# Block transposes of q and k on VectorE in place of TensorE transposes, in an attention and feed-forward kernel on one core

## The reference

```python
def _attn_ref(q, k, v, mem_k, mem_v):
    chunk, left_ctx, right_ctx = (32, 16, 8)
    scale = 1.0 / np.sqrt(D)
    for c in range(S // chunk):
        c_start = c * chunk
        c_end = c_start + chunk
        l_start = max(0, c_start - left_ctx)
        r_end = min(S, c_end + right_ctx)
        k_full = np.concatenate([mem_k, k[:, :, l_start:r_end]], axis=2)
        v_full = np.concatenate([mem_v, v[:, :, l_start:r_end]], axis=2)
        scores = scale * np.matmul(q[:, :, c_start:c_end], k_full.transpose(0, 1, 3, 2))
        scores = scores - np.max(scores, axis=-1, keepdims=True)
        a = np.exp(scores)
        a = a / (np.sum(a, axis=-1, keepdims=True) + 1e-09)
        out[:, :, c_start:c_end] = np.matmul(a, v_full)

def _moe_ref(x, w_in, w_out, g_ln):
    h = x @ w_in
    e = np.exp(h - np.max(h, axis=-1, keepdims=True))
    solu = h * e / (np.sum(e, axis=-1, keepdims=True) + 1e-09)
    ln = (solu - mean(solu)) / np.sqrt(var(solu) + 1e-06) * g_ln
    return ln @ w_out

def _moe2_ref(x, w_in, w_out):
    h = x @ w_in
    return (h * np.clip(h + 3.0, 0.0, 6.0) / 6.0) @ w_out
```

## Time and profile before

| | us |
|---|---|
| median of 3 runs | 904.52 |
| lowest, highest | 903.02, 905.22 |
| the profiled execution, its own time | 903.32 |
| its span, first to last instruction | 901.5 |
| mean granted TensorE clock | 0.992 |

### The profile page before, as it was taken

The page is one execution under the profiler, slowest core; times in us unless marked ns, Lnnn a source line. Parts: engine busy times, 40 slices in busy tenths (PEclk is TensorE's granted clock), DMA queues, the critical chain, the costliest instruction groups (busy, mean ns, idle before and its releaser), DMA issues.

```text
span 901.5 us, 18748 instructions
## 1 busy us (share of the span) xinstructions
PE 876.4 (97%) x7170; PEld 792.1 (88%) x7170; DVE 646.7 (72%) x1054; ACT 460.5 (51%) x1129; POOL 263.8 (29%) x308
## 2 busy tenths in 40 slices
PE   6899999999999999999999999999999999999998
PEld 5778988898888989899888888888799999999998
DVE  4768768787666778857685545554898887979784
ACT  5667555656565554537674555545754333333331
POOL 2474355465241453550122333223510000000000
PEclk8999999999999999999999999999999999999999
DMA  9965265554644474477733333333996434354341
GB/s 194 192 147 159 73 181 162 178 173 135 176 131 133 121 231 149 155 262 286 268 114 138 129 118 129 136 140 109 352 371 237 151 102 157 96 162 140 118 141 47
DMA packets 143496, 148.56 MB, mean 165 GB/s; under 512 B 91194, under 2 KB 102970, under 8 KB 142394
## 3 DMA queue, kind: packets, MB, share of 16 engines
q1 hardware_dynamic: 130272, 102.12, 37.3%
q0 software_dynamic: 7920, 38.94, 12.5%
q10 hardware_dynamic: 5226, 6.44, 2.2%
HBM read 89.92 MB, written 57.54 MB: 164 GB/s over the span
## 4 chain that ended last, share of the span: by engine, by line
PE 83%; DMA 5%; DVE 5%; ACT 3%; POOL 2%; issue 1%; SPq 1%; ACTq 0%; POOLq 0%; DVEq 0%
PE banks L1408 25%; PE banks L1147 25%; PE banks L1099 20%; PE banks L1114 3%; PE banks L1073 3%; PE banks L1044 2%; PE banks L991 2%; PE banks L1052 2%; PE banks L1090 2%; ACT prob L1497 1%; DMA xs_raw<-x_scratch 1%; POOL x_mix L897 1%; DMA x_mix<-x_scratch 1%; DMA x_mix_scratch<-x_mix 1%; DVE prob L1806 1%
## 5 line engine op out<-in xcount | busy, mean ns | idle before, releaser
L1408 PE MATMUL banks<-vs,gs 128*128 128x256 f32 x2016 | 242.8, 283 | 0.9 <-DMA vs<-v_split_scratch 0.8
L1408 PEld LDWEIGHTS banks<-vs,gs 128*128 128x128 f32 x2016 | 242.2, 192 | 1.6 <-DVE gs L1771 1.1
L1147 PE MATMUL banks<-xs,ws 128*128 128x512 f32 x1008 | 230.6, 390 | 0.5 <-ACT part L1550 0.2
L1147 PEld LDWEIGHTS banks<-xs,ws 128*128 128x128 f32 x1008 | 188.2, 188 | 41.6 <-issue 1.9
L1728 ACT CAST gs<-gs_raw 128x1792 fp32r<-128x1792 f32 x48 | 81.4, 1697 | 124.0 <-DVE gs_raw L2104 124.0
L1099 PE MATMUL banks<-y_t,w_out 128*128 128x384 f32 x768 | 141.1, 338 | 0.0
L1099 PEld LDWEIGHTS banks<-y_t,w_out 128*128 128x128 f32 x768 | 133.1, 188 | 0.8
L1099 PE MATMUL banks<-w_in,x_t 128*128 128x512 f32 x480 | 114.8, 395 | 1.1 <-DVE solu L1853 1.1
L1099 PEld LDWEIGHTS banks<-w_in,x_t 128*128 128x128 f32 x480 | 88.7, 188 | 19.9 <-DVE solu L1853 1.3
L2104 DVE TENSOR_TENSOR gs_raw<-gs_raw 128x256 f32<-128x256 f32 x192 | 82.2, 429 | 31.8 <-DMA gs_raw<-g_scratch 26.7
L1771 DVE TENSOR_TENSOR gs<-gs_raw,gs 128x1792 fp32r<-128x1792 f32 (+2 forms) x50 | 97.5, 1953 | 0.0
(11 more groups left out here) (104 smaller groups left out, 1012.7 us busy)
## 6 DMA issues: line engine op xcount, KB each, us to landing
g_scratch<-part SPq DMA_DIRECT2D x96, 256.0 KB, 2.0
gs_raw<-g_scratch SPq DMA_DIRECT2D x45, 512.0 KB, 4.0
x_scratch<-x_out ACTq DMA_DIRECT2D x32, 192.0 KB, 3.8
out_dram<-o_stage SPq DMA_DIRECT2D x11, 512.0 KB, 5.7
q_in<-in_q_dram SPq DMA_DIRECT2D x28, 192.0 KB, 3.0
v_split_scratch<-v_split POOLq DMA_DIRECT2D x3, 1792.0 KB, 7.6
ws<-w_split_scratch SPq DMA_DIRECT2D x21, 256.0 KB, 6.2
vs<-v_split_scratch SPq DMA_DIRECT2D x3, 1792.0 KB, 10.2
```

Source lines behind the costliest of these rows:

```text
L1147: mm = pe.matmul(ps, ws[:, W_OF[i], a, kc, :], xs[g][X_OF[i]][:, m, kc, :], start=(fresh and x == 0), stop=(x == len(passes) - 1), skip_gr ...
L1408: mm = pe.matmul(m_ps[i][:, s, :], gs[x][:, a, G_OF[i], s * P:(s + 1) * P], vs[p][:, m, V_OF[i], :], start=(p == 0 and s == 0 and y == 0), ...
```

## The change

Tiles 16 to 31 (batches 2 and 3) no longer have q and k turned by TensorE, and nothing is turned ahead in the first batch.

- **Relay.** While tiles 8 to 23 are worked on, SyncE issues eight DMAs a tile (`relay_step`), each from device memory to device memory. They put q and k of a group of four tiles into `q_blocks` and `k_blocks` so that each row of 128 partitions holds pieces of 32 floats of one 32-row chunk: 384 pieces of 128 bytes a DMA.
- **Loads.** A tile's q and k come from there, one DMA each, 384 bytes a run (`q_split`, `k_split`), behind a wait for the group's relay. In a batch's first tile twelve small DMAs bring the memory and left context rows as well.
- **VectorE.** `turn_blocks(n+1)` stands behind `norm_probs(n)`: three transposes of 32 by 32 squares (384, 256 and 128 columns), and one of 128 columns for `edge_t` in a batch's first tile. They write `q_t` and `k_t`.
- **ScalarE.** `join_blocks(n+1)` takes the place of the copies: three short copies within and between the k buffers, the second behind a wait for the first. The factor 1/8 moves into the exponential (`scale=SCALE`), whose bias is now `sbias`, one multiplication of the maxima per half tile, waited for.
- **TensorE.** The scores wait for `blocks_turned` and `qk_copied`; the probabilities' transposes of tiles 15 to 30 no longer wait for q and k copies.
- **GpSimd** waits for the first block's weights (`w_lo_done`) where it waited for `ahead_kept`.

```diff
-    AHEAD = 4
+    FIRST = 16
+    GROUP = 4
+    NQUAD = P // CHUNK
...
+        q_split = [at(f"q_split{s}", 136 + 2 * s, [P, KD, TQ], F32) for s in range(2)]
+        k_split = [at(f"k_split{s}", 140 + 2 * s, [P, KD, CHUNK + TQ], F32) for s in range(2)]
+        edge_t = at("edge_t", 162.5, [P, KD, CHUNK], F32)
+        sbias = at("sbias", 163, [TQ, H], F32)
...
             def load_q(b, t):
                 n = TILES * b + t
-                if n >= 2 and is_ahead(n - 2):
-                    sp.wait_ge(scores_done, 2 * n - 2)
+                if n >= 2 and by_blocks(n - 2):
+                    sp.wait_ge(blocks_turned, blocks_before(n - 2) + 1)
                 elif n >= 2:
                     sp.wait_ge(qk_turned, 2 * n - 3)
-                if is_ahead(n):
-                    sp.dma_start(q_back[t % 2][:, :, :], q_dram[n - NA + AHEAD]).then_inc(q_in_here[t % 2], 16)
+                if by_blocks(n):
+                    sp.wait_ge(relaid, relaid_count(n))
+                    sp.dma_start(q_split[t % 2][:, :, :], q_blocks[n // GROUP, :, :, n % GROUP * TQ:(n % GROUP + 1) * TQ]
+                                 ).then_inc(q_in_here[t % 2], 16)
                     return
...
+            def relay(g, part):
+                b, lo, x = GROUP * g // TILES, GROUP * TQ * g % S, part % KD
+                for dst, src, off in ((q_blocks, q, 0), (k_blocks, k, RIGHT)):
+                    e = part // KD
+                    head = (b * H + 2 * x + e // 2) * S + lo + off
+                    every = src.rearrange("b h s d -> (b h s) d")
+                    whole = min(GROUP * TQ, B * H * S - head) // CHUNK * CHUNK
+                    there = dst[g, CHUNK * e:CHUNK * (e + 1), x, :]
+                    cols = slice(CHUNK * (e % 2), CHUNK * (e % 2 + 1))
+                    sp.dma_start(there[:, 0:whole].rearrange("r (c d) -> r c d", d=CHUNK),
+                                 every[head:head + whole, cols].rearrange("(c r) d -> r c d", r=CHUNK)
+                                 ).then_inc(relaid, 16)
...
+            RELAY_STEPS = 4
+            PER_STEP = NQUAD * KD // RELAY_STEPS
+
+            def relay_step(n):
+                g = n // GROUP + 2
+                if FIRST // GROUP <= g < NA // GROUP:
+                    for part in range(n % GROUP * PER_STEP, (n % GROUP + 1) * PER_STEP):
+                        relay(g, part)
...
             first_batch()
-            pool.wait_ge(ahead_kept, 32 * AHEAD)
+            pool.wait_ge(w_lo_done, 2 * WP1)
             batch(1, steps=0, start=1)
...
-                if is_ahead(n):
+                if by_blocks(n):
                     return
...
             def scores(n, very_first):
-                if is_ahead(n):
-                    pe.wait_ge(q_in_here[n % 2], 16 * (n // 2 + 1))
-                    pe.wait_ge(k_in_here[n % 2], k_in_count(n))
-                    q_of, k_of = q_back[n % 2], k_back[n % 2]
-                else:
-                    pe.wait_ge(qk_copied, 2 * n + 2)
-                    q_of, k_of = q_t, k_t[n % 2 if n > TILES else 0]
+                if by_blocks(n):
+                    pe.wait_ge(blocks_turned, blocks_before(n + 1))
+                pe.wait_ge(qk_copied, 2 * n + 2)
+                q_of, k_of = q_t, k_t[n % 2 if n > TILES else 0]
...
+            def join_blocks(n):
+                new, old = k_t[n % 2], k_t[1 - n % 2]
+                act.wait_ge(blocks_turned, blocks_before(n + 1))
+                act.wait_ge(qk_copied, 2 * n)
+                memory, shared = (edge_t[:, :, 0:NMEM], edge_t[:, :, NMEM:CHUNK]) if n % TILES == 0 else \
+                    (old[:, :, MEM], old[:, :, NK - LEFT - RIGHT:NK])
+                nc.scalar.copy(new[:, :, 88:96], new[:, :, MEM]).then_inc(qk_copied, 1)
+                act.wait_ge(qk_copied, 2 * n + 1)
+                nc.scalar.copy(new[:, :, MEM], memory)
+                nc.scalar.copy(new[:, :, 0:LEFT + RIGHT], shared).then_inc(qk_copied, 1)
...
+                if by_blocks(n):
+                    hs = slice(HB * half, HB * (half + 1))
+                    nc.scalar.mul(sbias[:, hs], smax[:, hs], SCALE).then_inc(bias_done, 1)
+                    act.wait_ge(bias_done, 2 * (n - FIRST) + half + 1)
...
+            def turn_blocks(n):
+                s = n % 2
+                dve.wait_ge(q_in_here[s], 16 * (n // 2 + 1))
+                dve.wait_ge(scores_done, 2 * n)
+                nc.vector.transpose(q_t[:, :, :].rearrange("p h t -> p (h t)"),
+                                    q_split[s][:, :, :].rearrange("p h t -> p (h t)")).then_inc(blocks_turned, 1)
+                dve.wait_ge(k_in_here[s], k_in_count(n))
+                if n % TILES == 0:
+                    nc.vector.transpose(edge_t[:, :, :], k_split[s][:, :, 0:CHUNK]).then_inc(blocks_turned, 1)
+                nc.vector.transpose(k_t[s][:, :, 24:24 + 2 * CHUNK], k_split[s][:, :, CHUNK:3 * CHUNK]
+                                    ).then_inc(blocks_turned, 1)
+                nc.vector.transpose(k_t[s][:, :, NK - CHUNK:NK], k_split[s][:, :, 3 * CHUNK:]).then_inc(blocks_turned, 1)
...
                     if w["own"]:
                         norm_probs(n)
+                        if FIRST <= n + 1 < NA:
+                            turn_blocks(n + 1)
```

More of the change, by code:

```diff
@@ L360, in attention_solu_hardswish, with by_blocks, blocks_before, relaid_count @@
         IDENT_READY, THREE_READY, HALF_READY = 2, 3, 4
-        def is_ahead(n):
-            return n >= NA - AHEAD
-        def ahead_tile(e):
-            return TILES - AHEAD + e
-        def raw_count(e):
-            return 16 * (PIECES * (e // 2 + 1) + e // 2 + 2)
-        def is_joined(n):
-            return n >= TILES and n % TILES > 0 and not is_ahead(n)
+        def by_blocks(n):
+            return n >= FIRST
+        def blocks_before(n):
+            return sum(4 if x % TILES == 0 else 3 for x in range(FIRST, n))
+        def is_joined(n):
+            return TILES <= n < FIRST and n % TILES > 0
+        def relaid_count(n):
+            return 16 * sum(relay_parts(g) for g in range(FIRST // GROUP, n // GROUP + 1))
+        def relay_parts(g):
+            return 2 * NQUAD * KD + (4 if g == NA // GROUP - 1 else 0)
         def k_loads(n):
-            if is_ahead(n):
-                return 1
+            if by_blocks(n):
+                return 3 * NQUAD + 1 if n % TILES == 0 else 1
             return PIECES if is_joined(n) else window_loads(n // TILES, n % TILES)
@@ L508, in keep_ahead, with half_heads @@
[L508 to L511 removed]
+            def half_heads(src, e):
+                return src[e // 2::2, :, CHUNK * (e % 2):CHUNK * (e % 2 + 1)]
+            def relay(g, part):
[10 more added lines that the diff above has]
+                                 ).then_inc(relaid, 16)
+                    if whole < GROUP * TQ:
+                        left = CHUNK - RIGHT
+                        sp.dma_start(there[0:left, whole:], every[head + whole:, cols]).then_inc(relaid, 16)
+                        sp.dma_start(there[left:CHUNK, whole:], every[B * H * S - RIGHT:, cols]).then_inc(relaid, 16)
@@ L1057, in turn_probs @@
                 for half in range(2):
-                    if behind_qk and not is_ahead(n + 1):
+                    if behind_qk and not by_blocks(n + 1):
                         pe.wait_ge(qk_copied, 2 * n + 3 + half)
@@ L1671, in batch @@
                         high_x(n - 1, (kk - 2) % TPG, (kk - 2) // TPG % 2)
-                    if not last and not is_ahead(n + 1):
+                    if n + 1 < FIRST and not last:
                         copy_qk(n + 1)
+                    elif n + 1 < NA and not last:
+                        join_blocks(n + 1)
                     if w["mm1"]:
```

109 lines of the change are left out of this document (23 added, 86 removed).

## The result

| | before | after |
|---|---|---|
| median, us | 903.77 | **914.38** |
| lowest, highest | 902.86, 905.22 | 913.49, 916.23 |
| the profiled execution, its span | 903.32, 901.5 | 913.49, 911.7 |
| mean granted TensorE clock | 0.992 | 0.981 |

The ratio is 1.0123, with a 95% interval of 1.0104 to 1.0142: slower by 10.6 us. Four runs of each were compared. The prediction was 910.0 with a range of 899 to 922, slower with a chance of 0.58; the result lies inside the range, just above the band of 906 to 914 that it gave to its own mechanism.

The account below looks back on a forecast made before the run. TensorE, busy 97% of the span, was taken as the bound, except in short steps waiting for the probabilities. 903.3 - 7.2 gained + 9.9 waits + 3.8 clock = 909.8, given as 910.0, range 899 to 922.

Parts of the forecast that it names:

- rival 3: DMA queues: relay slower than they bear, beyond 38 ns a piece; +36 us at 50 ns, mostly 912 to 925; chance 0.15.
- first batch: First batch: 32 TensorE transposes of tiles turned ahead go, three groups on the chain; 1.1 us gained, bounds 0 and 2.6.
- nine ordinary steps: Ordinary steps among tiles 16 to 27: eight TensorE transposes each go, 0.66 us a step; 6.1 us gained.
- wait, tile 19: Short step of tile 19: scores wait for VectorE's transposes and ScalarE's join, so attention·V starts 2.6 us later.
- waits, tiles 23 and 27: Short steps of tiles 23 and 27: join ends at 271.05 instead of 269.68, +1.4 us each.
- wait, tile 31: Step of tile 31, not turned there before: two VectorE delays add up, attention·V at 371.2 instead of 366.68, +4.5 us.
- clock: TensorE behind the new stops: falls to 1.2 GHz, 2.5 of four at 1.5 us, +3.8 us; bounds 0 and 6.0.
- relay: DMA queues, tiles 8 to 23: 3072 pieces a step at 25 ns each, hidden, costing nothing.
- the four short steps: Tiles 19, 23, 27 and 31: no matmul work between transposes and scores, so new waits there sum to 9.9 us.
- rival 2: Faster: GpSimd's work falls elsewhere, transposes cost 0.6 us, no clock fall; 898.5, say 899; chance 0.18.
- N: Moment VectorE finishes a tile's probabilities; sets the short steps, where the next scores wait until 1.95 us after it.
- Rival 1: Short steps: waits without the clock's falls, or with one; 906 us; chance 0.22.

Follow-up runs that it names:

- experiment 1: Kernel before with the 132 relay DMAs added in the steps of tiles 8 to 23, read by nobody: 903.1 us, ratio 1.0023.
- experiment 2: Changed kernel with VectorE's transposes of tile n+1 moved ahead of the probabilities of tile n: 897.3 us, ratio 0.9949.
- experiment 6: Changed kernel with VectorE's transposes ahead of the probabilities and GpSimd's later split pieces waiting for tile 18's probabilities: 893.1 us, ratio 0.9869.
- experiment 9: The changed kernel run again, unaltered: 915.8 us, ratio 1.0140 to the kernel before.
- experiment 4: Changed kernel with nine useless 128 by 128 matmuls in each step of tiles 19, 23, 27, 31, and one `solu_done` wait: 906.5 us, ratio 1.0046.
- experiment 5: Changed kernel with GpSimd's two later weight-split pieces in tile 18's step held until tile 18's probabilities are done: 910.5 us, ratio 1.0072.
- experiment 8: Changed kernel with tiles 19, 23, 27 and 31 loaded as rows and turned by TensorE as before, relay left whole: 902.5 us, ratio 0.9988.

## Why the prediction was right, and where it was not

Forecast 910.0, measured 914.4: the direction and the mechanism were right, the size 4.4 us short. The forecast's own words give 1.2 us more than it says: its sum of 909.8 starts from the profiled execution, 1.2 us under the median, so 911.0 was meant. And part of the hit is luck: the width of the range above 914 had been given to a slow relay (rival 3), which did not come. From the profile of after, by the prediction's own steps:

| step | predicted | measured | where read |
|---|---|---|---|
| first batch | -1.1 | -2.1 | shift at tile 8; see below |
| nine ordinary steps | -6.1 | -5.5 | shifts; tiles 20 and 24, hidden by the clock, taken as 0.7 |
| wait, tile 19 | +2.6 | +4.3 | attention·V, less the shift of tile 18 and the clock |
| waits, tiles 23 and 27 | +1.4 each | +1.07 each | the same |
| wait, tile 31 | +4.5 | +3.9 | the same |
| clock | +3.8 | +6.8 | 2.7, 2.8, 1.3 and 0 at the four; see below |
| relay | 0 | 0 to 2 | experiment 1 |
| sum | +6.5 | +9.5 | second block starts 9.4 later (407.22 to 416.61) |

- **The prices were right.** VectorE's transposes 1.2 us (1.1 measured, 1.3 with the fourth of a batch's first tile; single ones 567, 398 and 265 ns), the join 0.7 (0.64 to 0.65), the products 0.20 each. The estimate from the Trainium skill ("VectorE: DVE Perf Modes", The three transpose paths), 1.9 us a tile by 311 ns for 128 columns of two-byte data, does not hold: 128 columns of four-byte data took 265 ns here. The Trainium skill's advice to use VectorE for 32 by 32 blocks (same page, Rules for kernel authors) holds on this kernel if they stand early enough (experiments 2 and 6), and not where the change put them.
- **The place of the loss was right.** The waits of the four short steps sum to 10.3 us against 9.9 predicted; at tiles 23 and 27 they were 0.3 shorter and at 31 0.6 shorter, which tile 19's excess of 1.7 more than made up. What was late next, the copies queued behind the join, came as said: 0.92 us at attention·V.
- **The term that was mis-sized is the clock.** I took 2.5 falls of 1.5 us. All four steps fell, and those of tiles 19 and 23 cost more than the one fall that the earlier trace rows showed. The fall at tile 31 delayed TensorE by 1.3 us as well; it counts 0 because before the change TensorE waited 1.14 us soon after it, for `solu` at 380.07, and no longer does. The second profile of the same kernel (experiment 9) has 9.5 us for the four, and holding the clock gained 8 us (experiment 4). Even the term's upper bound, 6.0, was too low: the 1.5 us came from a fall behind waits of 0.25 and 1.23 us, and the new waits are 2.7 to 5.0 us a step. Why one fall lasts longer than another is not shown.
- **The wait of tile 19** was 1.7 us too small, for the reason that stood in rival 2 with the other sign: GpSimd's work fell elsewhere, and onto the scaling that decides N. I had used that N moves with GpSimd as an argument for faster only. Experiment 5 takes away 2.6 us there, and 4 us in all.
- **Ordinary steps.** All gained 0.7 but tile 18's, which gained nothing. The prediction called VectorE's delay free there. What it overlooked is ScalarE, which waits for VectorE's transposes in the join, with the hidden exponential and the probability copies queued behind: attention·V behind the scores of tile 17 waited 0.85 us. VectorE was late in that step because a small instruction (L1791) took 1.80 us beside GpSimd's split; it did so before the change too, when nobody waited. With the transposes ahead (experiment 2) the step gained its 0.7. Experiment 8 shows the same wait at tile 30, larger.
- **The first batch** came out 2.1 us shorter in this profile, but experiment 1 shows 2.5 us without any edit there. Whether the 1.1 us were right stays open.
- **The relay.** I took 25 ns a piece, and 13.6 is measured; the conclusion (hidden) was the same. The Trainium skill ("DMA: Bandwidth & Descriptors", Specifications) has transfers below 512 bytes read, modify and write. Whether the engine does so no run here shows; the doubling that I worked out from it, 35 ns, is not seen. SyncE's issue was priced too low: 0.62 us in the median and up to 2.2, not 0.4; still it delayed no load that anyone waited for.
- **The rivals.** Rival 1 (waits without the clock, 906) is nearly what experiment 4 makes of the kernel: 906.5, though two stretches at the lower clock are left in it, so the closeness is partly chance. Rival 2 (faster) needed other causes than I gave it: not cheaper transposes but an earlier place.

## What to carry over

When an operation moves to another engine, ask first where in that engine's in-order stream its inputs are ready, and put it there: with the same three instructions the kernel was 11 us slower than before with them behind the probabilities and 5 us faster with them ahead. In the step where the bound engine has least to do, count the wait, what is queued behind it, and the slower clock after it; here holding the clock alone gave 8 us. Look for what GpSimd does beside the one VectorE instruction that everybody waits for, and move it if nobody is in a hurry for it.

## What the runs showed of the hardware that I had not expected

- VectorE's 32 by 32 transposes of four-byte data took 567 ns for 384 columns, 398 for 256 and 265 for 128: 1.0 to 1.3 ns for each further column.
- Pieces of 128 bytes from device memory to device memory took 13.6 ns of one DMA engine, less than the 256-byte pieces in the earlier trace rows (17.4).
- A scaling of 512 columns on VectorE took 0.69 us alone and 1.61 and 2.16 us beside GpSimd's splits, 1.65 beside its sums.
- Useless matmuls in the waits made the kernel 8 us faster (914.4 to 906.5), and with GpSimd moved as well 12 us.
- The same first batch differed by 2.5 us between two executions, with granted clocks of 0.91 and 1.00 from 45 to 65 us.
- In two executions of the same kernel the falls of the clock behind the same four waits cost 6.8 and 9.5 us.
